# Low halves of the first expert's weights: from GpSimd to VectorE, and an earlier load of the routing probabilities

## The reference

```python
scores = np.where((rel >= 0) & (rel < 64), scale * (q @ k.T), -1e9)
x = softmax(scores) @ v                      # 1152 x 512 after the heads are put side by side
p = domain_probs / (domain_probs.sum(-1, keepdims=True) + 1e-09)
for e in range(4):                           # w1[e]: 512 x 1024, w2[e]: 1024 x 512
    h = np.maximum(x @ w1[e], 0.0)
    out += p[:, e:e + 1] * (h @ w2[e])
# second mixture: rows with x @ w_skip > 0 go through the one of 8 experts with the highest logit,
# gated by its probability, and the result is added to x; the other rows stay as they are
```

## Time and profile before

| what | us |
|---|---|
| median of 3 runs | 686.45 |
| lowest, highest | 686.04, 686.49 |
| span of the profiled execution | 687.7 |
| TensorE busy in it | 638.3 (93%) |
| VectorE busy | 307.5 (45%) |
| ScalarE busy | 247.3 (36%) |
| GpSimd busy | 129.8 (19%) |

### The profile page before, as it was taken

One profiled execution on the slowest core, in us unless ns is written; L12 is line 12 of the kernel. 1 busy time (PEld: TensorE's weight loads), 2 busy tenths in 40 slices (PEclk: granted clock), 3 DMA queues, 4 the chain that ended last, 5 costly groups with the idle time before them and its releaser, 6 DMA issues. The chain is left out here.

```text
span 687.7 us, 9802 instructions
## 1 busy us (share of the span) xinstructions
PE 638.3 (93%) x3410; PEld 561.9 (82%) x3411; DVE 307.5 (45%) x784; ACT 247.3 (36%) x518; POOL 129.8 (19%) x166
## 2 busy tenths in 40 slices
PE   5589999999999999999999999999968999899883
PEld 4478989898989898989898989898856878678662
DVE  5866556624512133512133443455655364743740
ACT  5654445421402031302041312223335365734741
POOL 6340000000000000000000021211334365535441
PEclk9999999999999999999999999999998999999998
DMA  8722233104400003400003410424573563950830
GB/s 257 225 68 71 68 109 111 73 1 123 122 1 1 1 0 123 122 0 0 0 4 118 123 62 32 130 86 123 123 227 127 190 212 114 313 184 21 283 120 7
DMA packets 41409, 70.06 MB, mean 102 GB/s; under 512 B 13926, under 2 KB 18534, under 8 KB 41376
## 3 DMA queue, kind: packets, MB, share of 16 engines
q1 hardware_dynamic: 37040, 60.73, 28.8%
q0 software_dynamic: 4336, 8.91, 3.7%
HBM read 64.14 MB, written 8.47 MB: 106 GB/s over the span
## 5 line engine op out<-in xcount | busy, mean ns | idle before, releaser
L623 ACT ACTIVATE ht_hi<-ps_h 128x384 fp32r<-128x384 f32 (+1 forms) x104 | 48.6, 467 | 247.6 <-PE ps_h L1000 238.7
L1000 PE MATMUL ps_h<-xt_hi,w_hi_a 128*128 128x384 f32 (+1 forms) x400 | 132.3, 331 | 3.3 <-DVE ht_lo L815 3.3
L1000 PE MATMUL ps_h<-xt_hi,w_lo_a 128*128 128x384 f32 (+1 forms) x400 | 130.7, 327 | 0.0
L1000 PE MATMUL ps_h<-xt_lo,w_hi_a 128*128 128x384 f32 (+1 forms) x400 | 130.6, 327 | 0.0
L1000 PE MATMUL ps_y<-w_hi_a,ht_hi 128*128 128x512 f32 x288 | 117.2, 407 | 0.0
L1000 PE MATMUL ps_y<-w_lo_a,ht_hi 128*128 128x512 f32 x288 | 114.1, 396 | 0.0
L1000 PE MATMUL ps_y<-w_hi_a,ht_lo 128*128 128x512 f32 x288 | 114.0, 396 | 0.0
L815 DVE SCALAR_TENSOR_TENSOR ht_lo<-ps_h,ht_hi 128x384 fp32r<-128x384 f32 (+1 forms) x104 | 54.7, 527 | 120.3 <-ACT ht_hi L623 120.0
L1000 PEld LDWEIGHTS ps_h<-xt_hi,w_hi_a 128*128 128x128 f32 x400 | 75.2, 188 | 4.3 <-DVE ht_lo L815 3.9
L709 DVE TENSOR_TENSOR w_lo_a<-raw,w_hi_a 128x1024 fp32r<-128x1024 f32 x56 | 68.3, 1243 | 17.6 <-ACT w_hi_a L558 17.6
L1000 PEld LDWEIGHTS ps_h<-xt_lo,w_hi_a 128*128 128x128 f32 x400 | 75.2, 188 | 0.4
(11 more groups left out here) (156 smaller groups left out, 862.9 us busy)
## 6 DMA issues: line engine op xcount, KB each, us to landing
raw<-u SPq DMA_DIRECT2D x64, 512.0 KB
raw<-w SPq DMA_DIRECT2D x32, 512.0 KB
vt<-v SPq DMA_DIRECT2D x17, 256.0 KB, 2.9
kt<-k SPq DMA_DIRECT2D x8, 384.0 KB, 5.1
qz<-q SPq DMA_DIRECT2D x18, 128.0 KB, 3.9
x_rows<-x POOLq DMA_DIRECT2D x9, 256.0 KB, 4.8
out<-x POOLq DMA_DIRECT2D x9, 256.0 KB
kt<-k SPq DMA_DIRECT2D x1, 256.0 KB, 3.8
```

Of the source, the lines that this page charges most:

```text
L623: a.activation(ht_hi[:, pos, 0:P * tiles], ps_h[:, pos % 2, 0:P * tiles], ACT.Relu).then_inc(h_hi_done, 1)
L1000: ins = mm(dst, hi_lo[l], rhs_hi_lo[r], start=(first and n == 0), stop=(last and n == 2))
```

## The change

GpSimd's loop over the eight low halves is taken out. VectorE makes the four of w1 in the prologue, after its steps 3, 4, 6 and 8, each one step behind ScalarE's high half. It makes the four of w2 in the first chunk of the first expert, at positions 1, 3, 4 and 6, each one position behind ScalarE's high half and behind the ht_lo of that position. The load of the probabilities is issued third by SyncE, behind keys 0 and values 0 and ahead of keys 1, instead of behind values 3.

```diff
@@ weight_pieces
             for i, pos in enumerate((0, 2, 3, 5)):
-                at[pos] = [("first_weights", KC + i)]
+                at.setdefault(pos, []).append(("first_weights", KC + i))
+                at.setdefault(pos + 1, []).append(("first_lo", KC + i))
@@ block.sync
             load_keys(0)
             load_values(0)
+            sp.dma_start(probs_e[:], dp).then_inc(p_landed, 16)
             load_keys(1)
             weights(w1, 0, pieces=(0, 1))
...
             load_values(3)
-            sp.dma_start(probs_e[:], dp).then_inc(p_landed, 16)
@@ block.gpsimd
-            for i in range(CHUNK_W):
-                j = i % KC
-                if i < KC:
-                    hi_done, split, hi, lo = w1_hi_done, w1_split, w1_hi[0][:, j, :], w1_lo[0][:, j, :]
-                else:
-                    hi_done, split = w2_hi_done, w2_split
-                    hi, lo = (w[0][:, 2 * j:2 * j + 2, :].rearrange("p j d -> p (j d)") for w in (w2_hi, w2_lo))
-                pool.wait_ge(hi_done, j + 1)
-                g.tensor_tensor(lo, raw[:, j, :], hi.bitcast(F32), ALU.subtract).then_inc(split, 1)
@@ block.vector, beside
+                    elif what[0] == "first_lo":
+                        weights_lo(0, what[1], 0)
@@ block.vector, prologue
             for p in range(PROLOGUE):
                 attention(p)
+                if p - 3 in PROLOGUE_PIECES:
+                    weights_lo(0, PROLOGUE_PIECES.index(p - 3), 0)
             dve.wait_ge(p_landed, 16)
```

More of the change, by code:

```diff
@@ L47, in build_block @@
     NPAIR = NT * PAIRS
-    CHUNK_W = 2 * KC
     RING = 4
```

## The result

The changed kernel takes 689.84 us in the median of 22 runs (685.47 to 694.24), the kernel before 687.2 in 22 runs (684.45 to 692.09): a ratio of 1.0044, with a 95% interval of 1.0025 to 1.0063. The forecast was 684.6. The number behind +- is the standard error. Both kernels scatter over 8 to 9 us, far more than the three runs of before that the forecast started from, so the ratio needs the experiments beside it.

The account below looks back on a forecast made before the run. TensorE, busy 93% of the span, was the bound, with time to win only in the first 53 us. Second product at 34.55 + 16.3 = 50.8 against 52.62, so 686.45 - 1.85 = 684.6 us; range 682.8 to 686.9.

Parts of the forecast that it names:

- The slow small operations: VectorE's small operations in prologue and first chunk: slow while GpSimd makes low halves, six excesses of 11.3 us in all.
- The 9.9 us of low halves: Eight low halves added to VectorE: 9.9 us busy time against 11.3 taken away, so its load stays.
- Both of TensorE's stops: First chunk: TensorE's waits of 1.85 and 1.45 us for a ht_lo of VectorE would go.
- the one before the second product: End of first chunk: TensorE idle some 0.65 us, waiting for the last low half on VectorE.
- a pair of steps: Attention steps ahead of the first chunk: each of the next two pairs takes 5.8 us, low half included.
- The early load: Probabilities' load ahead of the second keys on SyncE's queue: delays what follows by 0 to 0.43 us, taken as 0.35.
- 15.48 us is work: First chunk: of TensorE's 18.78 us from first block to second product, 3.30 is idle and 15.48 work.
- the sum 15.48 + 0.8 = 16.3: First chunk after the change: work plus 0.8 us idle, so the second product begins at 50.8 against 52.62.
- the clock among the rivals: Routed experts: a fall of TensorE's clock, 1.7 us each, added or lost; chance 0.13 of one more, 0.04 of two.
- The forecast's first block, 34.55: TensorE's start of the first expert: 33.84 before, plus 0.4 for the chain and 0.35 for the early load.
- The chance given to "slower": Whole kernel: 0.12, from half of rival VectorE-bound (0.14), two clock falls (0.04), VectorE staying slow (0.02) and a little more.
- 1.4 us for what a measurement can tell from no change: Whole kernel: about 0.2%; the chance of a result within it was put at 0.28.

Follow-up runs that it names:

- e9: Kernel before, cut off behind the first expert (other dense experts and all routing left out): mean 177.26 +- 0.44 us in 6 runs.
- e13: Kernel before, unchanged to the byte, run again: 685.05 us median, ratio 0.9929 to the runs of the kernel before beside it.
- e5: Kernel before with 8 extra matmuls before each wait for gathered rows in the routed experts (busy tail): 695.8 us median.
- e8: Kernel before with extra matmuls in the prologue (8, 2, 8, 2, 8 in attention steps 6 to 10): 687.55 us median, ratio 1.0002.
- e3: Kernel before with only the load of the probabilities moved ahead of the second keys: 686.69 us, ratio 0.996.
- e12: Kernel before with only the early load of the probabilities, cut off behind the first expert: mean 175.96 +- 0.58 us in 6 runs.
- e1: Changed kernel with extra matmuls in the prologue (8, 2, 8, 2, 8 in attention steps 6 to 10): 685.24 us median, ratio to before 0.9963.
- e16: Changed kernel with three low halves of w1 in front of the wait for xt_hi, plus extra prologue matmuls (5, 2, 5, 2, 8): 681.26 us median, ratio 0.9871.
- e4: Changed kernel, unchanged, run again beside the kernel before: 688.07 us median, ratio to before 0.9985.
- e6: Changed kernel with 8 extra matmuls before each wait for gathered rows in the routed experts (busy tail): 696.7 us median.
- e10: Changed kernel, cut off behind the first expert: mean 177.46 +- 0.33 us in 5 runs.
- e14: Changed kernel, unchanged, run a third time beside the kernel before: 687.97 us median, ratio 0.9996.
- e2: Changed kernel with the load of the probabilities back behind values 3, so the low halves alone: 688.68 us median, ratio 1.001.
- e7: Changed kernel with extra matmuls both in the prologue and before each wait for gathered rows: 693.18 us median.
- e11: Changed kernel with extra matmuls in the prologue, cut off behind the first expert: mean 175.44 +- 0.42 us in 5 runs.
- e15: Changed kernel with the second to fourth low half of w1 in front of the wait for xt_hi, not behind it: 682.95 us median, ratio 0.9899.

## Why the prediction was wrong

**What held.** The slow small operations are GpSimd's doing: with its pieces gone every pair of multiplications takes 0.48. The 9.9 us of low halves measured 9.8, and VectorE's load did not rise. Both of TensorE's stops are gone, and the one before the second product is 0.63 (forecast 0.65). The chunk took 16.05 us at the high clock, against my 16.3. From the first high half to the first block I had 21.55 us; the profiles of the changed kernel have 22.25 to 22.91, since a pair of steps takes 6.06 and not 5.8 (18.92 to 24.98 and on to 31.04 in the profile after). The early load cost the first weights nothing that can be seen: 12.38 against 12.65.

**The step that failed** is "15.48 us is work", and the sum 15.48 + 0.8 = 16.3 from it. It took the durations of one execution for the work itself. In that execution TensorE's clock had risen by 22 us and stayed up, which is seldom: of the six runs of e9 one, at 0.990, came near it, and e9, e13 and e5 have a low clock in the prologue or at the first block. With a fall across the first block the chunk of the changed kernel takes longer, by 1.3 to 2.75 us (17.35 to 18.80 in place of 16.05, eight profiles). The kernel before has 18.2 to 19.2 with a fall or without one, because a fall also takes its first stop away. So the gain of the chunk was real and was given back in the same microseconds. The forecast set 16.3 against 18.78; with a fall in both kernels, 17.35 to 18.80 stands against 18.2:

| second product minus first block, us | no fall in the chunk | a fall across the first block |
|---|---|---|
| kernel before | 18.78 (first profile), 18.79 (e5, up again when the block starts), 19.20 (e8) | 18.24 (e9), 18.21 (e13); with the early load 18.22 (e3), 18.23 (e12) |
| changed kernel | 16.05 (e1, e16) | 18.32, 17.35 (e4), 18.33 (e6), 18.80 (e10), 18.80 (e14); 17.42 (e2), 17.60 (e7), 17.62 (e11) |

I had the clock among the rivals, but in the tail alone. In the prologue the windows from 0 to 20 us show 1.00 although four matmuls took 1.06 us there and 0.61 from 22 us on. In e13 the windows show 1.00 up to 35 us, and four matmuls take 1.06 up to 28. In these profiles the column reads 1.00 until the first fall that it records. I read that column and not the durations. What the rows show at a fall: in the profile of after, the granted clock goes to 0.50 near 22.9 and 33.1 us (the windows of 22 and 33 have 0.94 and 0.56), 2.2 and 0.3 us after TensorE had begun again behind waits of 2.79 and 2.23 us. The Trainium skill, TensorE: Matmul & The Clock Gate, section HAM oscillation — how this bites in real kernels, says of short bursts of matmuls with waits for transfers between them that the next burst starts cold. The trace agrees only in part: the waits here are for ScalarE, the first burst began at the high clock, and in the profile of before no fall followed waits of up to 1.85 us.

The forecast's first block, 34.55, was early by 0.3 on average (34.13 to 35.37, mean 34.87 in the five profiles). The chance given to "slower" adds up to 0.13 from its three parts, not 0.12.

**The sign.** The measured slowdown of 0.44% is not explained by this stretch. The starts of the second product average 53.2 in five profiles of the changed kernel (after, e4, e6, e10, e14) and 53.3 in four of the kernel before (before, e5, e9, e13), and the cut kernels are equal. The other two comparisons of the full kernel gave 0.9985 and 0.9996. Over all runs the means are 689.10 +- 0.45 (46 runs) and 687.56 +- 0.26 (126), 1.5 us apart (688.77 and 687.18); e13 shows that a ratio of 0.7% can come between two sets of runs of one program. Whether a part of it belongs to the change, behind the first expert, stays open: the busy tail, which was to decide it, gave 0.8 +- 1.4, and what makes a wait end in a fall in one execution and not in the next was not found. What is shown is that the change gains nothing in the first expert, and why.

**The size of chance.** I took 1.4 us for what a measurement can tell from no change, from three runs within 0.45 us. The 22 runs of the same kernel go from 684.45 to 692.09. The rival of the tail named the source, and its size per fall (1.7), but gave it 0.17 in all; with two profiles of one kernel 5.5 us apart in the routed experts it deserved most of the range.

## What to carry to other kernels

Time taken from TensorE's waits is only won if TensorE's clock is up when it is given back. And before counting a stop as a gain, look at a second profile: a slow stretch of one engine can move another engine's work, and with it the stop, as in e9. Read the durations of one kind of matmul before and after every wait, not the clock column alone. And put movable work in front of an engine's own wait, not behind it: with the same three low halves in front of the wait for xt_hi the first block started 3.1 us earlier (31.81 in e15 against 34.87 in the mean of five profiles), and 4.0 earlier with the extra matmuls (30.61 in e16 against 34.63 in e1).

## What was not expected of the hardware

TensorE's clock in a thin prologue is a matter of the single execution: in the kernel before it stayed up from 22 us on in one profile, was at 0.50 from 18 to 34 us in another (e5), and in a third (e13) was low by the durations until 28 us, rose, and was at 0.50 again from 36 to 39. 22 extra matmuls held it in e16, and 28 of them in e1 from 20 us on, but not in e7 and e11, where it was at 0.50 for about 3 us from 35 or 36 on. And one run of e7 took 3186 us, all others of it between 688.72 and 696.28; nothing in the profiles says why.
